# FFT filter and two MLPs on one core: ten products of a cleared tile at the start, first input pieces over two queues, two first-stage copies on ScalarE, another order in slot 1

## The reference

```
Y = irfft(rfft(x, axis=1) * (filt_r + 1j * filt_i))    # x: 2 x 3008 x 256
h = Y @ w_in ;  z = maximum(0.01 * h, h) @ w_out       # 256 -> 2048 -> 256
h = z @ w_in2 ; r = maximum(h, 0) ; out = (r * r) @ w_out2
```

## Time and profile before

| | us |
|---|---|
| median of 3 runs | 1096.76 |
| lowest and highest run | 1095.6, 1096.91 |
| profiled execution, its own time | 1096.96 |
| span from its first to its last instruction | 1094.9 |
| PE busy | 1084.5 |
| VectorE, ScalarE, GpSimd busy | 772.5, 566.9, 292.7 |

### The profile page before, as it was taken

How to read it: one execution, slowest core, us unless ns; L and a number is a source line. 1 busy time by engine, 2 the same in 40 slices (tenths; PEclk the granted TensorE clock), 3 DMA queues, 4 the chain that set the end, 5 groups by cost and what they waited for, 6 DMA issues and landing times.

```text
span 1094.9 us, 14037 instructions
## 1 busy us (share of the span) xinstructions
PE 1084.5 (99%) x5088; PEld 912.1 (83%) x5088; DVE 772.5 (71%) x1185; ACT 566.9 (52%) x981; POOL 292.7 (27%) x285
## 2 busy tenths in 40 slices
PE   8999999999999999999999999999999999999998
PEld 8778888888888888888888888888888888888887
DVE  2997788776677677667666766766676667667665
ACT  3456655554565455555554554554554554554543
POOL 0688254134234324323220120120220220220000
PEclk9999999999999999999999999999999999999999
DMA  8778500012212112112244200100100000000000
GB/s 302 216 221 260 176 1 1 22 43 54 48 44 58 44 44 58 44 44 54 81 132 156 73 1 1 40 1 1 39 1 1 37 1 1 39 1 1 39 1 36
DMA packets 70340, 66.08 MB, mean 60 GB/s; under 512 B 40832, under 2 KB 56192, under 8 KB 70272
## 3 DMA queue, kind: packets, MB, share of 16 engines
q1 hardware_dynamic: 69984, 64.99, 19.3%
q10 hardware_dynamic: 288, 0.20, 0.1%
HBM read 41.19 MB, written 23.99 MB: 60 GB/s over the span
## 4 chain that ended last, share of the span: by engine, by line
PE 97%; DVE 2%; DMA 0%; issue 0%; POOL 0%; ACT 0%; SPq 0%; DVEq 0%
PE PS L947 16%; PE PS L946 16%; PE PS L948 16%; PE PS L954 14%; PE PS L955 14%; PE PS L956 14%; PE PS L898 2%; PE PS L888 2%; PE PS L861 2%; PE PS L916 1%; PE PS L877 1%; DMA X<-in_x 0%; DVE YL L750 0%; DVE YT L728 0%; DVE XF L721 0%
## 5 line engine op out<-in xcount | busy, mean ns | idle before, releaser
L636 ACT ACTIVATE GH<-GF 128x512 fp32r<-128x512 f32 (+1 forms) x384 | 238.7, 622 | 225.8 <-DVE GF L810 116.4
L816 DVE TENSOR_TENSOR GL<-GF,GH 128x512 fp32r<-128x512 f32 (+1 forms) x384 | 258.4, 680 | 106.4 <-ACT GH L636 100.2
L947 PE MATMUL PS<-GL,WOH 128*128 128x512 f32 (+1 forms) x768 | 296.3, 386 | 0.0
L946 PE MATMUL PS<-GH,WOH 128*128 128x512 f32 (+1 forms) x768 | 296.3, 386 | 0.0
L948 PE MATMUL PS<-GH,WOL 128*128 128x512 f32 (+1 forms) x768 | 296.1, 386 | 0.0
L954 PE MATMUL PS<-XH,WIH 128*128 128x512 f32 (+1 forms) x672 | 260.0, 387 | 1.2 <-DVE GF L801 1.2
L956 PE MATMUL PS<-XH,WIL 128*128 128x512 f32 (+1 forms) x672 | 259.2, 386 | 0.0
L784 DVE TENSOR_TENSOR GF<-PS,GF 128x512 f32<-128x512 f32 (+1 forms) x96 | 65.3, 680 | 167.2 <-ACT GF L607 167.2
L948 PEld LDWEIGHTS PS<-GH,WOL 128*128 128x128 f32 x768 | 144.1, 188 | 27.7
L946 PEld LDWEIGHTS PS<-GH,WOH 128*128 128x128 f32 x768 | 144.2, 188 | 27.6
L947 PEld LDWEIGHTS PS<-GL,WOH 128*128 128x128 f32 x768 | 144.1, 188 | 27.6
(11 more groups left out here) (70 smaller groups left out, 954.4 us busy)
## 6 DMA issues: line engine op xcount, KB each, us to landing
zu<-U SPq DMA_DIRECT2D x32, 192.0 KB, 3.0
V<-zu SPq DMA_DIRECT2D x12, 512.0 KB, 5.2
FL<-in_filt SPq DMA_DIRECT2D x16, 336.0 KB, 4.3
X<-in_x SPq DMA_DIRECT2D x8, 512.0 KB, 8.4
out_y<-YT SPq DMA_DIRECT2D x4, 1024.0 KB, 4.3
wi<-PWH SPq DMA_DIRECT2D x16, 224.0 KB, 2.5
wi<-PWL SPq DMA_DIRECT2D x16, 224.0 KB, 3.1
WIH<-wi SPq DMA_DIRECT2D x8, 448.0 KB, 3.5
```

The source lines that it names most:

```text
L636: nc.scalar.activation(GH[:, g, 0:width(s)], GF[:, g, 0:width(s)], ACT.Copy).then_inc(g_hi[kind], 1)
L816: nc.vector.tensor_tensor(GL[:, g, 0:w], GF[:, g, 0:w], GH[:, g, 0:w].bitcast(f32), ALU.subtract).then_inc(g_lo[kind], 1)
L946: nc.tensor.matmul(acc, wh, xh, start=first, stop=False)
L947: nc.tensor.matmul(acc, wh, xl, start=False, stop=False)
```

## The change

Four things change. VectorE first clears a tile `WARM` (128 x 128 float32, in space that is unused until slot 0), and PE starts with ten products of that tile with itself, whose result nobody reads. The input is cut into pieces of 2, 2, 2, 2, 4, 4, 4, 4 rows, and pieces 1 and 3 of batch 0 are issued by ScalarE between the two table loads, while SP issues the others in their order (pieces 0, 2, 4 first). Half 1 of chunks 10 and 11 is copied by ScalarE (`n1_copy_late`), and the clearing of the pad of `XF` waits for half 1 of chunk 9 in place of the first `spectrum`. In slot 1 alone, VectorE's `g_split(0, UB)` comes behind `whole_a(1)` and `whole_c(0)`.

```diff
-XG = (1, 1, 2, 2, 2, 4, 4, 4, 4)
+XG = (2, 2, 2, 2, 4, 4, 4, 4)
+    WARM = at("WARM", [128, 128], f32, o_s)
+        X_BY_ACT = ((0, 1), (0, 3))
@@ sync, load_x
-                    sp.dma_start(X[:, b, m:m + n, :], ...).then_inc(x_in[b][g], 16)
+                    if (b, g) not in X_BY_ACT:
+                        sp.dma_start(X[:, b, m:m + n, :], ...).then_inc(x_in[b][g], 16)
@@ gpsimd
-            pool.wait_ge(p_ps, 1)
+            pool.wait_ge(n1_ps[1], CH - LATE + 2)
             nc.gpsimd.memset(XF[32:IM, :, :, :], 0.0).then_inc(xf_pad, 1)
@@ scalar
             act.dma_start(DM[:, 0, :], dft[:, 0, :]).then_inc(dft_in, 16)
+            for b, g in X_BY_ACT:
+                m, n = X_START[g], XG[g]
+                act.dma_start(X[:, b, m:m + n, :], x[:, b, m:m + n, :]).then_inc(x_in[b][g], 16)
             act.dma_start(DM[:, 1:3, :], dft[:, 1:3, :]).then_inc(dft_rest, 16)
...
-            for i in range(3):
-                turned(i)
+            turned(0)
+            turned(1)
+            n1_copy_late(CH - 2)
+            turned(2)
+            n1_copy_late(CH - 1)
@@ vector
-            for c in range(CH - LATE):
+            nc.vector.memset(WARM[:, :], 0.0).then_inc(warm_sb, 1)
+            for c in range(CH - 2):
                 n1_copy(c)
-            n1_copy(CH - LATE)
-            for i in range(2):
-                n1_copy(CH - LATE + 1 + i)
-                filtered(i)
-            n1_copy(CH - 1)
+            filtered(0)
+            filtered(1)
...
                 if s >= 1:
                     g_act(s - 1, UB)
+                if s >= 2:
                     g_split(s - 1, UB)
                 if s < SLOTS:
                     whole_a(s)
                 if s >= 1:
                     whole_c(s - 1)
+                if s == 1:
+                    g_split(0, UB)
@@ tensor
+            pe.wait_ge(warm_sb, 1)
+            for _ in range(10):
+                nc.tensor.matmul(PS[:, 0, 0:128], WARM[:, :], WARM[:, :], start=True, stop=True)
             pe.wait_ge(dft_in, 16)
...
-                    pe.wait_ge(n1_sb[1], CH)
+                    pe.wait_ge(n1_sb[1], CH - 2)
+                    pe.wait_ge(n1_late, 2)
```

More of the change, by code:

```diff
@@ L98, in fft_mlp_kernel @@
         n1_sb = [sem("n1_sb_act"), sem("n1_sb_dve")]
+        n1_late = sem("n1_late")
+        warm_sb = sem("warm_sb")
         ft_in = [sem(f"ft_in{g}") for g in range(FSLOTS)]
@@ L208, in load_x @@
             def load_x(b):
-                m = 0
                 for g, n in enumerate(XG):
-                    sp.dma_start(X[:, b, m:m + n, :], x[:, b, m:m + n, :]).then_inc(x_in[b][g], 16)
-                    m += n
+                    m = X_START[g]
+                    if (b, g) not in X_BY_ACT:
+                        sp.dma_start(X[:, b, m:m + n, :], x[:, b, m:m + n, :]).then_inc(x_in[b][g], 16)
             def load_filter(f):
@@ L575, in x_round, with n1_copy_late @@
                     nc.scalar.activation(XH[x][:, 6, 0:w], XT[x][:, 2, 0:w], ACT.Copy).then_inc(xf_hi, 1)
-            for i in range(3):
-                turned(i)
+            def n1_copy_late(c):
+                act.wait_ge(n1_ps[1], c + 1)
+                nc.scalar.activation(n1_out(c, 1), PS[:, 6 + c % 2, :].rearrange("p (m q) -> p q m", m=4), ACT.Copy).then_inc(n1_late, 1)
+            turned(0)
[3 more added lines that the diff above has]
+            n1_copy_late(CH - 1)
             for i in range(UNITS):
```

## The result

| | before | changed |
|---|---|---|
| median, us (8 runs each) | 1096.87 | 1093.22 |
| lowest and highest, us | 1095.6, 1098.03 | 1092.54, 1094.08 |
| profiled execution, us | 1096.96 | 1092.61 |
| its span, us | 1094.9 | 1090.8 |

The ratio of the changed kernel's time to that of the kernel before is 0.9967, with a 95% interval of 0.9956 to 0.9978: 2.4 to 4.8 us faster. The forecast was 1092.4 us, a gain of 4.4 us; by the medians the gain is 3.65 us.

A forecast was written before the change was run, and what follows sets the result against it. PE, holding 97% of the chain of waits, bounds the kernel, losing time at the start, the seam and slot 1. Gains of 2.65 + 0.87 + 0.87 = 4.39 us from 1096.76 give 1092.4 us, range 1091.0 to 1094.7.

The forecast's parts named there:

- Part 3: Slot 1: PE's 1.16 us wait for `whole_c(0)` vanishes, a snapshot wait at `group_c(1)` follows; gain 0.87 us, bounds 0.5 and 1.2.
- Part 2: Seam to stage two: without VectorE's two copies and its clearing wait, `inverse(2)` no longer waits; gain 0.87 us, bounds 0.5 to 0.95.
- Part 1: Start: after ten products stage one begins at 5.3 us, transposes at 24.7; gain 2.65 us, bounds 0.5 and 3.4.
- The rise of the clock: Start: PE goes from 213 to 111 ns between 5.3 and 7.0 us, putting the transposes at 24.3 to 25.1.
- The products of zeros: Start, a rival: zeros don't raise the clock, it rises at 11.3 us; 1094.6 us in all, chance 9%.
- the rival of the early rise: Start: the clock rises before stage one begins; gain 3.05 to 3.4 + 1.74, 1091.6 to 1092.0 us; chance 23%.
- Nothing there is late: Start: piece 0 lands between 3.4 and 5.0 us, piece 1 between 3.9 and 5.5, wanted at 5.8 or later.
- the bound of 0.3 us on the waits for input: Start: piece 4 of batch 0, wanted at 9.3 us, makes PE wait 0 to 0.3 us.
- The sentence that gave the second queue no credit: Start: issuing input from ScalarE too is worth nothing beyond about 0.45 us of issue; the sum gives it nothing.
- if PE waits for `X`: Start, closing sign: the forecast is wrong if PE waits for input, or if spacing stays 213 ns beyond 8 us.
- The rival with a late piece: Start: piece 1 waits behind SP's backlog and PE stands; slower if landing from 7.2 us on, 1099 at 9.5; chance 4%.
- Its formula: Start: if the late piece lands at L and the clock is down again, the transposes come at L + 21.9 us.

The follow-up runs named there:

- new pieces alone: The kernel before with the new input pieces, 1 and 3 of batch 0 on ScalarE, and nothing else: 1095.84 us, ratio 0.9999.
- no products, tables behind: Changed without the ten products, only piece 1 on ScalarE, stage two's tables issued after the last input piece landed: 1093.02 us, ratio 0.9965.
- the kernel with the old copies: Changed, but the two late copies are VectorE's again, between the units; the early clearing stays: 1093.45 us, ratio 0.9972.

## Why the prediction was right, and where it was off

**Part 3** was forecast at 0.87 us, with 1.16 us won and the snapshot as the next wait. Both are in the trace; PE's weight load for `group_c(1)` waits 0.42 us for the snapshot. The term measures 1.1 us (bounds 0.5 to 1.2). The snapshot starts 4.78 us behind `whole_b(0)` (123.29 to 128.07), where the step had 4.9. The rest is that the step compared with the weight load of before, at 132.72: in an unbroken stream that load runs 0.22 us ahead of its product (132.94), while after the wait both start together at 128.70.

**Part 2** was forecast at 0.87 us and measures 0.88 to 0.89. `inverse(2)` was said to come 11.4 us behind the transposes with no idle time: 11.44. The ScalarE copy for unit 3 starts at 31.90, 6.50 us behind the transposes against 6.44 before, so it was covered. The step said rightly that the gain stops at 0.87 us because PE is then full. It did not say that the edits overlap: the copies alone give all of it and the clearing alone 0.62 us.

**Part 1** is the term that was mis-sized: 2.65 us forecast, 1.94 in the trace. Its pieces:
- The start of PE at 1.0 us and of stage one at 5.3: 1.06 and 5.18. Right.
- The rise of the clock: forecast in the middle between 5.3 and 7.0 us. In the ten traces with products it rose between 4.8 and 7.2 us, in seven of them by 5.9. I take that from the distances between the starts of PE's instructions, which fall from 213 to 111 ns. In the changed kernel it was at 4.8 us; in the kernel with all pieces on SP at about 6.8 us, and the count of PE's instructions (those over an edge counted twice) goes from x7 to x11:

```profile
5.00:6.00 1.00, 1.00 (x7) 1.00 1.07 266
6.00:7.00 1.00, 1.00 (x7) 1.00 0.87 332
7.00:8.00 1.00, 1.00 (x11) 1.00 1.02 406
```

The Trainium skill, "TensorE: Matmul & The Clock Gate", Part 1, says that the point varies from run to run, and these traces agree. The products of zeros do count towards the rise: in all ten traces it came at most 1.7 us after the first product of stage one and by 7.2 us, while in the four traces without products it came 3.2 us or more after that, at 7.2, 7.6, 9.9 and 12.1 us. In the profiled execution the rival of the early rise is what happened.
- The step that failed is "Nothing there is late". It worked out when pieces 0 and 1 land, and piece 4, and passed over piece 3, the second on ScalarE's queue. That one landed at 8.7 us where PE wanted it at 7.4, and took 1.13 us back; the bound of 0.3 us on the waits for input was too narrow. The sentence that gave the second queue no credit was right, but it did not ask whether that queue could cost something. By the prediction's own last words, "if PE waits for `X`", part 1 went wrong here.
- The rival with a late piece named the right queue and the wrong piece: piece 1 landed at 5.1 us, before it was wanted. Its formula would put the transposes at 8.7 + 21.9 = 30.6 us; they came at 25.4, since 20 of the 168 instructions were done by then and the clock was not down again: behind the wait, 148 instructions take 16.85 us.
- A second limit stood behind it and was not seen: the tail of the input. The last piece landed at 22.9 us instead of 20.9. In this trace that cost nothing, since PE ran unbroken from 8.71 us, but it held PE up in two others. The tables, asked for at 17.56 instead of 19.50 while input is still in flight, are part of the reason and not the whole of it (see above). The forecast looked at who wants the tables and not at what they run into.

With an early rise (3.05 us) and a wait of 1.13 us the working of part 1 gives 1.92 us, against 1.94 measured. The terms add: 1.94 + 0.89 + 1.11 = 3.94, and 0.18 us between them that no step had.

That the sum of 4.39 us came so near to the 4.12 of the traces is partly luck. The late piece took 1.13 us that no term had; an early rise (0.40), slot 1 (0.24) and the 0.18 us that belong to no step gave most of it back.

**What was not settled.** By the runs the ten products are worth 1.7 to 2.1 us alone and 1.05 us where nothing else stops stage one, but nothing that shows in the changed kernel itself, where the late piece hides them. What the new pieces are worth alone lies between nothing and 1 us. Why piece 3 lands between 8.3 and 9.7 us on ScalarE's queue, and why a late 512 KB piece sometimes lags, is open.

## What to carry to other kernels

- When an edit makes an engine ready sooner, list every transfer that it will want in the new order with its landing, not only the first and the largest: here the one piece that was left out took 1.1 of 3 us.
- A transfer on a second issuing engine's queue need not be served in the order in which it is wanted. Here piece 3 landed at 8.3 to 9.7 us on ScalarE's queue and at 6.8 to 7.8 on SP's, and the medians were 0.6 to 0.7 us lower with it on SP. Keeping what is needed next in one queue, in order of need, lost nothing.
- Two edits that both shorten the work of an engine ahead of a full PE need not add up: here 0.62 and 0.88 us gave 0.88. Undo each alone before you credit it.

## What the runs showed of the hardware

- The level of PE's clock cannot be read from the granted clock in these profiles: it says 1.00 where instructions come every 213 ns and where they come every 111 ns. The distance between starts tells it. From the beginning of PE's work to the rise it took 3.8 to 6.1 us in the ten traces with products. Without them it took 3.2 us (no products), 3.6 us (new pieces alone), 5.9 us (no products, tables behind) and 6.1 us (before, from the end of its pause).
- A wait of 1.66 us after the rise did not bring the clock down: in the kernel with the old copies PE waited that long for piece 3, and from the second instruction behind the wait on the starts were 111 ns apart.
- A 256 KB piece issued at 1.66 us on ScalarE's queue landed after a 512 KB piece issued at 1.65 us on SP's: 8.7 against 8.5 us.
- The kernels with the products have a time that lies 1.7 to 1.9 us above their span in every run. For those without (the kernel before, no products, no products with tables behind, new pieces alone) it is 1.7 to 3.2 us. Part of what the products bring may thus lie outside the span; no row shows where.
